# Unit loads ahead of the decay rows' loads, and the first expert's weights split inside the attention units

## The chip, the cores and the metric

The kernel runs on one core of a Trainium2 chip, in one launch. The metric is the device time of that core in microseconds. It is float32 throughout; the large products are made from pairs of rounded halves ("hi" and "lo", type fp32r).

## The reference

Three stages follow each other. B, H, S, D are 2, 8, 768, 40, so that there are 1536 tokens of 320 features.

```python
# 1. gated linear attention, a recurrence over t
m_new = max(f[t] + m, i[t])
f_stab, i_stab = exp(f[t] + m - m_new), exp(i[t] - m_new)
C = f_stab * C + i_stab * outer(v[t], k[t])      # state per batch and head
n = f_stab * n + i_stab * k[t]
y[t] = sigmoid(o[t]) * (C @ q[t]) / max(abs(n . q[t]), 1)
# 2. four dense experts, weights [320, 1024] and [1024, 320]
out += p[:, e] * (relu(x @ w1[e]) @ w2[e])
# 3. eight routed experts, the top one for each token, capacity 384
out[tok] = gate[tok] * (relu(x[tok] @ w1[e]) @ w2[e])
```

## The kernel before

**Attention.** The recurrence is cut into chunks of 128 tokens. A *unit* is one chunk of one batch (8 heads); there are 12, numbered u = 0 to 11, and they alternate between the two batches. For a unit PE (TensorE) makes, in this order: the scores (L445), the first half of the next unit's decay rows spread over 128 partitions (`spread_g`, L432), the products with the carried state (L455), the update of the state (L463), the transposes of the output of unit u-2 (L481), the first three heads' products with v (L473), the second half of the spread (L432), and the other heads' products (L473). ACT (ScalarE) turns the spread rows into `dmat` by Exp (`decays`, L705). POOL (GpSimd) masks a corner of `dmat` (`mask`, L892), weighs v for the next unit (L902), carries the state (`carry_state`, L909), scales the output gate (`scale_o`, L930) and adds up the new state (L918). DVE (VectorE) multiplies scores by `dmat` (`pmat`, L1067), takes the denominator of the unit before (L1103 to L1107), scales `before` (L1077), makes `state_new` (L1083), `x_tok` (L1112) and `xt_lo` (L1118), and at the end `total` (L1095). The order on each engine is written out in the code; semaphores join them.

Waits that matter here: `pmat` of unit u waits for `masked` >= u+1, which POOL's `mask(u)` raises. PE's products with the state of unit u+1 wait for `comb_done`, which DVE's `total` of unit u raises. `scale_o` waits for the reciprocal of the denominator, and `x_tok` for `scale_o`.

**Loads.** SP (SyncE) issues nearly all DMAs, in program order. `load_unit` issues five for a unit: three into `q_diag` (60 KB each), one into `qk_rows` (360 KB) and one into `kv` (324 KB), into four sets of buffers; the load of unit u waits for `in_ready` >= u-3. `load_g` issues one of 8 KB, the decay rows of a unit, two of its partitions only, into two buffers; it waits for `g_spread`, that is until PE has spread the rows of unit u-2.

**Experts' weights.** An expert comes in four pieces p of 704 KB (`load_piece`) into `stage`. ACT rounds a piece into `w1_hi` and `w2_hi` (`w_to_hi`, parts 0 and 1, L737 and L740), DVE makes a shared tail (`w_tail`, L1126), and POOL takes the rests (`w1_to_lo`, L872, which waits for `w_tail`; `w2_to_lo`, L880, which waits for `w_to_hi` part 1). A block of 384 tokens is `up` (L507 to L510) and `down` (L522 to L524). Before, the first expert's piece 0 is loaded after unit 3's load and pieces 1 to 3 after the last unit's; its splitting starts around unit 11 and goes on beside the first block. There `w1_first` and `w_ready` let PE start on the pieces as they are ready.

Of the kernel before, what the change touches and what calls it, by code (L numbers as in the profile page):

```python
# [41 lines left out]
def build_kernel(nc, gates, o_tok, q_t, qk_t, kv_tok, probs, w_moe1, w_moe2, w_gate, out, capacity):  # L42
# [40 lines left out]

    W_STEPS = (1, 3, 5, 7)

    SHIFTED, CHOSEN, SLOTS = 2, 5, 14
# [13 lines left out]
    with ExitStack() as ctx:  # L100
# [174 lines left out]
        w_tail_done = sem("w_tail_done")  # L275
        w1_first = sem("w1_first")
        w_ready = sem("w_ready")
# [30 lines left out]
        def _(sp):  # L308
# [24 lines left out]
            sp.wait_ge(pool_const, CONST_DIAG)  # L333
            load_unit(0, 0)
            sp.wait_ge(g_lo_done, 1)
            sp.dma_start(g_dram.rearrange("n h s -> h n s"), g_split[:].bitcast(F32)).then_inc(g_saved, 16)
            sp.wait_ge(g_saved, 16)
            for b in range(BATCHES):
                sp.wait_ge(mask_rows, b + 1)
                load_g(0, b)  # L340
            load_unit(0, 1)


            for u in range(2, 4):
                sp.wait_ge(g_spread, 2 * (u - 1))
                load_g(u // 2, u % 2)
                load_unit(0, u)
            for p in range(1):
                load_piece(w_moe1, 0, p)
            with sp.Fori(1, UNITS // 4) as i:  # L350
                for j in range(4):
                    sp.wait_ge(in_ready, 4 * i + (j - 3))
                    load_unit(i, j)
                    sp.wait_ge(g_spread, 8 * i + (2 * j - 2))
                    load_g(2 * i + j // 2, j % 2)
            for p in range(1, PIECES):
                load_piece(w_moe1, 0, p)

# [40 lines left out]
        def _(pe):  # L399
# [129 lines left out]
            def first_weights_there(f):  # L529
                if f in LAST_X:  # L530
                    transpose_x(UNITS // 4 - 1, 2 + LAST_X.index(f))
                if f % 2 == 0:
                    pe.wait_ge(w1_first, f // 2 + 1)

            def first_w2_there(n, f):
                if n == 0 and f % 2 == 0:
                    pe.wait_ge(w_ready, f // 2 + 1)
            pe.wait_ge(xt_done, (NT - 1) * BATCHES + 2)
            up(0, 0, lambda k: xt_hi[:, k, 0:BLOCK], lambda k: xt_lo[:, k, 0:BLOCK], first_weights_there)
            down(0, 0, first_w2_there)  # L540

# [141 lines left out]
        def _(act):  # L683
# [40 lines left out]
            decays(0, 2)  # L724
            with act.Fori(0, UNITS // 4 - 1) as i:
                for r in range(2, 6):
                    x_tail(i, r - 2)
                    decays(i, r + 1, [0])
                    x_to_hi(i, r - 2)
                    decays(i, r + 1, [1])  # L730

# [14 lines left out]

            def first_to_hi(p):
                w_to_hi(0, 0, p, 0)
                w_to_hi(0, 0, p, 1)


            i = UNITS // 4 - 1
            x_tail(i, 0)
            decays(i, 3, [0])
            x_to_hi(i, 0)
            decays(i, 3, [1])
            first_to_hi(0)
            x_tail(i, 1)
            x_to_hi(i, 1)
            first_to_hi(1)  # L760
            first_to_hi(2)
            x_tail(i, 2)
            first_to_hi(3)

# [13 lines left out]
            for e in range(E1 - 1):  # L778
                for c in range(BLOCKS1):
                    for f in range(FT):  # L780
                        hidden_hi(BLOCKS1 * e + c, f)

                        if f in ((2, 5) if e or c else (5, 6)):
                            w_to_hi(e + 1, (e + 1) % 2, c, f // 4 if e or c else f - 5)
                        if e == 0 and c == 0:
                            if f + 1 in LAST_X:
                                x_to_hi(UNITS // 4 - 1, 2 + LAST_X.index(f + 1))
                            if f == 1:
                                x_tail(UNITS // 4 - 1, 3)
# [39 lines left out]
        def _(pool):  # L829
# [102 lines left out]


            for u in range(UNITS - BATCHES):
                if u + 1 < UNITS - BATCHES:
                    weigh_v(u + 1)
                    carry_state(u + 1)
                if u:
                    scale_o(u - 1)
                mask(u + 1)  # L940
                new_state(u)
            scale_o(UNITS - 3)
            mask(UNITS - 1)

            for p in range(PIECES):
                w1_to_lo(0, 0, p).then_inc(w1_first, 1)
                if p < 2:
                    scale_o(UNITS - 2 + p)
            for p in range(PIECES):
                w2_to_lo(0, 0, p)  # L950

# [60 lines left out]
        def _(dve):  # L1012
# [133 lines left out]
            attend(0, 1)  # L1146
            with dve.Fori(0, UNITS // 4 - 1) as i:
                for r in range(2, 6):
                    attend(i, r)
            i = UNITS // 4 - 1  # L1150
            attend(i, 2, last_chunk=True)
            w_tail(0, 0, 0, slice(0, PF))
            attend(i, 3, last_chunk=True)
            denominator(i, 3)
            w_tail(0, 0, 1, slice(PF, 2 * PF))
            w_tail(0, 0, 2, slice(2 * PF, 3 * PF))
            w_tail(0, 0, 3, slice(3 * PF, 4 * PF))

# [16 lines left out]
            for f in range(FT):  # L1175
# [3 lines left out]
                if f == 0:  # L1179
                    make_x(UNITS // 4 - 1, 3)  # L1180
                if f == 6:
                    w_tail(1, 1, 0, slice(0, PF))
# [193 lines left out]
```

## Time and profile before

| | |
|---|---|
| median of 3 runs | 634.91 us (634.17 to 637.78) |
| span of the profiled execution, first to last instruction | 634.1 us |
| mean granted TensorE clock over the span | 0.982 |
| PE busy | 588.4 us (93%), 3842 matmuls |
| DVE busy | 285.8 us (45%) |
| ACT busy | 215.3 us (34%) |
| POOL busy | 212.4 us (33%) |

The profiled execution's own time is its span of 634.1 us and what lies around it, 0.8 us if it is like the median run. PE is busy nearly all the time, so the time of the whole is made by PE's work and by the few stretches in which PE has none. Attention's units lie between 23 and 93 us of the span, the first block of the first expert between 93 and 117 us. An engine's low share says nothing about a stage: DVE is busy 45% of the whole, but most of the time in the units.

### The profile page before, as it was taken

To read this page: it belongs to the slowest core of one execution; us is meant where nothing else is said; L and a number is where in the kernel's file an instruction comes from. 1 tells how busy PE (TensorE), PEld (TensorE's weight loads), DVE (VectorE), ACT (ScalarE), POOL (GpSimd) and SP (SyncE) were. 2 spreads that over 40 slices of the span, in tenths; PEclk is the share of its full clock that TensorE was granted. 3 is DMA by queue.
4 is the path that set the end of the run, shared out by engine and by line. 5 is a ranking of instruction groups with operands and counts; after the bars stand their busy time and mean duration, and the time that the engine had idled before them with its cause. 6 is when DMAs were issued, how large, how long until landed. Compare 5 with 4: busy or idle time off the path is not lost.

```text
span 634.1 us, 10634 instructions
## 1 busy us (share of the span) xinstructions
PE 588.4 (93%) x3842; PEld 573.1 (90%) x3842; DVE 285.8 (45%) x607; ACT 215.3 (34%) x468; POOL 212.4 (33%) x238
## 2 busy tenths in 40 slices
PE   0989999999999999999999999999889398899995
PEld 0868889999999999999999999999889398899895
DVE  7268876323332332233223324244425089866362
ACT  5235564212321331133123213214115077646330
POOL 9555539101101110111011011231216157874451
PEclk9999999999999999999999999999979799999999
DMA  6487534941101101110111011120144347774300
GB/s 188 119 207 181 155 152 139 369 190 46 33 12 47 45 3 42 45 47 0 45 45 45 1 47 47 38 81 12 76 141 147 105 136 229 255 231 154 118 15 18
DMA packets 25914, 63.56 MB, mean 100 GB/s; under 512 B 3310, under 2 KB 15543, under 8 KB 25876
## 3 DMA queue, kind: packets, MB, share of 16 engines
q1 hardware_dynamic: 23956, 58.98, 29.3%
q0 software_dynamic: 1920, 4.07, 1.8%
q8 instruction: 25, 0.41, 0.3%
q14 instruction: 13, 0.11, 0.1%
HBM read 52.16 MB, written 13.11 MB: 103 GB/s over the span
## 4 chain that ended last, share of the span: by engine, by line
PE 84%; issue 5%; POOL 3%; DMA 3%; SPq 1%; DVE 1%; ACT 1%; POOLq 0%; DVEq 0%; ACTq 0%
PE bank L507 28%; PE bank L522 12%; PE bank L523 12%; PE bank L524 12%; PE bank L510 5%; PE bank L509 5%; PE bank L445 3%; PE bank L473 2%; DMA g_rows<-g_saved_rows 1%; PE bank L577 1%; PE bank L432 1%; PE bank L636 1%; PE bank L455 1%; PE bank L463 1%; SPq L315 1%
## 5 line engine op out<-in xcount | busy, mean ns | idle before, releaser
L745 ACT ACTIVATE h_hi<-bank 128x384 fp32r<-128x384 f32 x192 | 94.4, 492 | 324.0 <-PE bank L510 323.7
L1161 DVE SCALAR_TENSOR_TENSOR h_lo<-bank,h_hi 128x384 fp32r<-128x384 f32 x192 | 105.5, 556 | 143.4 <-ACT h_hi L745 141.3
L522 PE MATMUL bank<-w_hi_even,h_hi 128*128 128x320 f32 x264 | 81.7, 309 | 0.0
L524 PE MATMUL bank<-w_hi_even,h_lo 128*128 128x320 f32 x264 | 81.6, 309 | 0.0
L523 PE MATMUL bank<-w_lo_even,h_hi 128*128 128x320 f32 x264 | 81.5, 309 | 0.0
L872 POOL TENSOR_TENSOR w_lo_odd<-stage,w_hi_odd 128x512 fp32r<-128x512 f32 x24 | 31.3, 1304 | 149.2 <-DVE w_hi_odd L1126 119.6
L872 POOL TENSOR_TENSOR w_lo_even<-stage,w_hi_even 128x512 fp32r<-128x512 f32 x24 | 31.4, 1308 | 144.2 <-DVE w_hi_even L1126 119.6
L522 PE MATMUL bank<-w_hi_odd,h_hi 128*128 128x320 f32 x248 | 77.4, 312 | 1.4 <-DVE h_lo L1161 1.4
L523 PE MATMUL bank<-w_lo_odd,h_hi 128*128 128x320 f32 x248 | 76.6, 309 | 0.0
L524 PE MATMUL bank<-w_hi_odd,h_lo 128*128 128x320 f32 x248 | 76.6, 309 | 0.0
L507 PE MATMUL bank<-xt_hi,w_hi_odd 128*128 128x384 f32 (+2 forms) x192 | 64.3, 335 | 10.4 <-issue 10.4
L507 PE MATMUL bank<-xt_hi,w_hi_even 128*128 (+2 forms) x192 | 65.2, 339 | 4.8 <-DVE h_lo L1161 1.9
L507 PE MATMUL bank<-xt_lo,w_hi_even 128*128 (+2 forms) x192 | 63.3, 330 | 0.0
L507 PE MATMUL bank<-xt_hi,w_lo_even 128*128 (+2 forms) x192 | 63.2, 329 | 0.0
L1170 DVE SCALAR_TENSOR_TENSOR acc<-bank,prob,acc 128x320 f32 (+1 forms) x36 | 19.8, 551 | 95.8 <-PE bank L524 92.9
L507 PE MATMUL bank<-xt_lo,w_hi_odd 128*128 128x384 f32 (+2 forms) x192 | 62.3, 325 | 0.0
L507 PE MATMUL bank<-xt_hi,w_lo_odd 128*128 128x384 f32 (+2 forms) x192 | 62.3, 324 | 0.0
L522 PEld LDWEIGHTS bank<-w_hi_even,h_hi 128*128 128x128 f32 x264 | 49.6, 188 | 0.3 <-DVE h_lo L1161 0.3
L524 PEld LDWEIGHTS bank<-w_hi_even,h_lo 128*128 128x128 f32 x264 | 49.6, 188 | 0.0
L523 PEld LDWEIGHTS bank<-w_lo_even,h_hi 128*128 128x128 f32 x264 | 49.6, 188 | 0.0
L522 PEld LDWEIGHTS bank<-w_hi_odd,h_hi 128*128 128x128 f32 x248 | 46.6, 188 | 1.7 <-DVE h_lo L1161 1.7
L523 PEld LDWEIGHTS bank<-w_lo_odd,h_hi 128*128 128x128 f32 x248 | 46.6, 188 | 0.0
(162 smaller groups left out, 1165.8 us busy)
## 6 DMA issues: line engine op xcount, KB each, us to landing
stage<-w_moe SPq DMA_DIRECT2D x48, 704.0 KB, 4.0
slot_rows<-empty_row SPq DMA_DIRECT2D x1, 4632.0 KB, 20.0
x_slot<-slot_rows SPq DMA_DIRECT2D x24, 193.0 KB, 3.9
qk_rows<-qk_t SPq DMA_DIRECT2D x12, 360.0 KB
kv<-kv_tok SPq DMA_DIRECT2D x12, 324.0 KB
q_diag<-q_t SPq DMA_DIRECT2D x36, 60.0 KB
sig<-o_tok SPq DMA_DIRECT2D x2, 960.0 KB, 6.8
out<-empty_row SPq DMA_DIRECT2D x2, 960.0 KB, 18.6
```

What stands on the lines that cost most here:

```text
L445: pe.matmul(ps_s[g][:, lo:IN_GROUP * P], qk_rows[j][:, 1, g, :], q_diag[j][:, g, lo:], start=True, stop=True).then_inc(s_ready, 1)
L473: mm = pe.matmul(ps_in[:, h * V1:(h + 1) * V1], pmat[:, h, :], v41[j][:, h, :], start=True, stop=True)
L507: pe.matmul(dst, wk[w][:, k, cols], xk(k), start=(n == 0), stop=False)
L509: pe.matmul(dst, w1_hi[w][:, 2, cols], xh(2), start=False, stop=False)
L510: pe.matmul(dst, w1_hi[w][:, 2, cols], xl(2), start=False, stop=True).then_inc(h_psum, 1)
L522: pe.matmul(ps_y[n][:, 0:X], h_hi[:, f, rows], w2_hi[w][:, f, :], start=(f == 0), stop=False)
L523: pe.matmul(ps_y[n][:, 0:X], h_hi[:, f, rows], w2_lo[w][:, f, :], start=False, stop=False)
L524: mm = pe.matmul(ps_y[n][:, 0:X], h_lo[:, f, rows], w2_hi[w][:, f, :], start=False, stop=(f == FT - 1))
L745: act.activation(h_hi[:, f, :], ps_h[f % 3][:, 0:BLOCK], ACT.Relu).then_inc(h_hi_done, 1)
L872: return pool.tensor_tensor(w1_lo[w][:, :, cols], raw1[:, 0:2, :], w1_hi[w][:, 0:2, cols].bitcast(F32), ALU.subtract)
L1161: dve.scalar_tensor_tensor(h_lo[:, f, :], ps_h[f % 3][:, 0:BLOCK], 0.0, h_hi[:, f, :].bitcast(F32), ALU.max, ALU.subtract).then_inc(h_done, 1)
L1170: op = dve.scalar_tensor_tensor(acc[:, tile, 0:X], ps_y[n][:, 0:X], share, acc[:, tile, 0:X], ALU.mult, ALU.add)
```

## The change

SP's loads of the first four units move ahead of the decay rows' loads. The loop over the other units is written out, and a piece of the first expert is loaded behind the decay rows of units 4, 5, 6 and 7. In the units from 4 on, ACT rounds one part of a piece per unit, DVE makes a piece's tail behind each even unit, and POOL takes one rest per unit: w1's in the even ones, w2's in the odd ones. `w1_first` is gone; PE waits for `w_ready` alone. For the second expert, ACT rounds its first piece behind tiles 2 and 5 of the first block, not behind 5 and 6.

```diff
 (SP)
-            load_unit(0, 0)
+            for j in range(2):
+                load_unit(0, j)
             sp.wait_ge(g_lo_done, 1)
...
                 load_g(0, b)
-            load_unit(0, 1)
+            for j in range(2, 4):
+                load_unit(0, j)
             for u in range(2, 4):
                 sp.wait_ge(g_spread, 2 * (u - 1))
                 load_g(u // 2, u % 2)
-                load_unit(0, u)
-            for p in range(1):
-                load_piece(w_moe1, 0, p)
...
+            for u in range(4, UNITS):
+                sp.wait_ge(in_ready, u - 3)
+                load_unit(u // 4, u % 4)
+                sp.wait_ge(g_spread, 2 * (u - 1))
+                load_g(u // 2, u % 2)
+                if u >= FIRST_W and u < FIRST_W + PIECES:
+                    load_piece(w_moe1, 0, u - FIRST_W)
 (ACT)
+            for u in range(2, UNITS - 1):
+                x_tail(0, u - 2)
+                decays(0, u + 1, [0])
+                x_to_hi(0, u - 2)
+                decays(0, u + 1, [1])
+                if u >= FIRST_W:
+                    w_to_hi(0, 0, (u - FIRST_W) // 2, (u - FIRST_W) % 2)
...
+            w_to_hi(0, 0, PIECES - 1, 1)
             x_tail(i, 2)
-            first_to_hi(3)
 (POOL)
                 if u:
                     scale_o(u - 1)
+                if u >= FIRST_W:
+                    first_to_lo(u - FIRST_W)
                 mask(u + 1)
                 new_state(u)
             scale_o(UNITS - 3)
+            first_to_lo(UNITS - 2 - FIRST_W)
             mask(UNITS - 1)
-            for p in range(PIECES):
-                w1_to_lo(0, 0, p).then_inc(w1_first, 1)
-                if p < 2:
-                    scale_o(UNITS - 2 + p)
-            for p in range(PIECES):
-                w2_to_lo(0, 0, p)
+            first_to_lo(UNITS - 1 - FIRST_W)
+            scale_o(UNITS - 2)
+            scale_o(UNITS - 1)
 (DVE)
+            for u in range(2, UNITS):
+                attend(0, u, last_chunk=u >= UNITS - BATCHES)
+                if u >= FIRST_W and u % 2 == 0:
+                    p = (u - FIRST_W) // 2
+                    w_tail(0, 0, p, slice(p * PF, (p + 1) * PF))
```

The order on SP, from the first unit's load to the load of unit 4, before. `g_saved_rows` is where the decay rows lie in DRAM.

```order
L315 DMA q_diag<-q_t 40x3x128 x3
L316 DMA qk_rows<-qk_t 120x768
L317 DMA kv<-kv_tok 128x648
L321 DMA g_rows<-g_saved_rows 2x8x128 [waits g_spread]
L315 DMA q_diag<-q_t 40x3x128 x3
L316 DMA qk_rows<-qk_t 120x768
L317 DMA kv<-kv_tok 128x648
L324 DMA stage<-w_moe 128x1408
```

These rows are unit 2's load, the decay rows of unit 3, unit 3's load and the first piece; unit 4's load follows. The same place after:

```order
L316 DMA q_diag<-q_t 40x3x128 x3
L317 DMA qk_rows<-qk_t 120x768
L318 DMA kv<-kv_tok 128x648
L322 DMA g_rows<-g_saved_rows 2x8x128 [waits g_spread] x2
L316 DMA q_diag<-q_t 40x3x128 [waits in_ready]
L316 DMA q_diag<-q_t 40x3x128 x2
L317 DMA qk_rows<-qk_t 120x768
L318 DMA kv<-kv_tok 128x648
L322 DMA g_rows<-g_saved_rows 2x8x128 [waits g_spread]
L325 DMA stage<-w_moe 128x1408
```

Unit 3's load now stands ahead of the decay rows of units 2 and 3, and the first piece behind the load and the decay rows of unit 4.

The order on POOL in a unit, before; `dmat` in the fourth row is the mask of the next unit.

```order
L902 TENSOR_TENSOR vw<-kv,cols 128x328 [waits upd_ready,unit_in1]
L909 TENSOR_TENSOR state_kept<-state,c_all 120x369 [waits state_done]
L930 TENSOR_TENSOR osc<-sig,rden 128x320 [waits x_main,rden_done]
L892 AFFINE_SELECT dmat<-dmat 2x8x2 [waits exp_done]
L918 TENSOR_TENSOR state<-state_new,state_kept 120x369 [waits state_step,state_carried]
```

And after, in units 4 and 5:

```order
L888 TENSOR_TENSOR vw<-kv,cols 128x328 [waits upd_ready,unit_in1]
L895 TENSOR_TENSOR state_kept<-state,c_all 120x369 [waits state_done]
L916 TENSOR_TENSOR osc<-sig,rden 128x320 [waits x_main,rden_done]
L858 TENSOR_TENSOR w_lo_even<-stage,w_hi_even 128x2x256 [waits w_tail_done]
L878 AFFINE_SELECT dmat<-dmat 2x8x2 [waits exp_done]
L904 TENSOR_TENSOR state<-state_new,state_kept 120x369 [waits state_step,state_carried]
L888 TENSOR_TENSOR vw<-kv,cols 128x328 [waits upd_ready,unit_in2]
L895 TENSOR_TENSOR state_kept<-state,c_all 120x369 [waits state_done]
L916 TENSOR_TENSOR osc<-sig,rden 128x320 [waits x_main,rden_done]
L866 TENSOR_TENSOR w_lo_even<-stage,w_hi_even 128x640 [waits w_hi_done]
L878 AFFINE_SELECT dmat<-dmat 2x8x2 [waits exp_done]
```

A rest of the weights now stands between `scale_o` and the next unit's mask. The last rows of POOL's part in attention, before and after:

```order
L892 AFFINE_SELECT dmat<-dmat 2x8x2 [waits exp_done]
L872 TENSOR_TENSOR w_lo_even<-stage,w_hi_even 128x2x256 [waits w_tail_done]
L930 TENSOR_TENSOR osc<-sig,rden 128x320 [waits x_main,rden_done]
L872 TENSOR_TENSOR w_lo_even<-stage,w_hi_even 128x2x256 [waits w_tail_done]
L930 TENSOR_TENSOR osc<-sig,rden 128x320 [waits x_main,rden_done]
L872 TENSOR_TENSOR w_lo_even<-stage,w_hi_even 128x2x256 [waits w_tail_done] x2
L880 TENSOR_TENSOR w_lo_even<-stage,w_hi_even 128x640 [waits w_hi_done] x4
```

Behind unit 11's mask there were four rests of w1 and four of w2. After:

```order
L916 TENSOR_TENSOR osc<-sig,rden 128x320 [waits x_main,rden_done]
L858 TENSOR_TENSOR w_lo_even<-stage,w_hi_even 128x2x256 [waits w_tail_done]
L878 AFFINE_SELECT dmat<-dmat 2x8x2 [waits exp_done]
L866 TENSOR_TENSOR w_lo_even<-stage,w_hi_even 128x640 [waits w_hi_done]
L916 TENSOR_TENSOR osc<-sig,rden 128x320 [waits x_main,rden_done] x2
```

Now the last rest of w1 stands ahead of unit 11's mask, and one rest of w2 behind it.

## Rows read from the trace of the kernel before

**Rows 1.** The page: the span, and TensorE's busy time.

```profile
span 634.1 us, 10634 instructions
PE 588.4 (93%) x3842; PEld 573.1 (90%) x3842; DVE 285.8 (45%) x607; ACT 215.3 (34%) x468; POOL 212.4 (33%) x238
```

**Rows 2.** Timeline, PE: scores of units 3, 4, 10, 11 (start, duration in us).

```profile
41.75 1.97 PE L445 MATMUL bank<-q_diag,qk_rows 120*128 120x384 f32 x6
...
50.44 1.97 PE L445 MATMUL bank<-q_diag,qk_rows 120*128 120x384 f32 x6
...
84.02 1.97 PE L445 MATMUL bank<-q_diag,qk_rows 120*128 120x384 f32 x6
...
88.95 1.97 PE L445 MATMUL bank<-q_diag,qk_rows 120*128 120x384 f32 x6
```

**Rows 3.** Chain that ended last, 36 to 52 us: start, duration, what.

```profile
39.06 7.36 DMA g_rows<-g_saved_rows
46.42 0.12 issue
46.54 0.50 PE bank L432
```

**Rows 4.** Timeline, SP: when DMAs are issued.

```profile
24.70 0.28 SPq L321 DMA_DIRECT2D g_rows<-g_saved_rows  x1
...
34.12 0.43 SPq L324 DMA_DIRECT2D stage<-w_moe  x1
...
34.92 2.74 SPq L315 DMA_DIRECT2D q_diag<-q_t  x3
...
38.43 0.36 SPq L317 DMA_DIRECT2D kv<-kv_tok  x1
```

**Rows 5.** Timeline, PE and POOL in unit 8.

```profile
73.30 0.23 POOL L892 TENSOR_SCALAR_AFFINE_SELECT dmat<-dmat 2x16 f32<-2x16 f32 x1 [1.70 <-ACT dmat L705]
...
74.86 0.79 PE L455 MATMUL bank<-state,qk_rows 120*128 120x123 f32 x6
75.14 0.79 POOL L909 TENSOR_TENSOR state_kept<-state,c_all 120x369 f32<-120x369 f32 x1
...
76.48 0.76 PE L473 MATMUL bank<-kv,pmat 128*128 128x41 f32 x6
```

**Rows 6.** Timeline, DVE in unit 8: `pmat`, `den`, `total`.

```profile
73.75 1.53 DVE L1067 TENSOR_TENSOR pmat<-bank,dmat 128x384 f32<-128x384 f32 x3 [0.22 <-PE bank L445]
...
75.20 0.76 DVE L1103 SCALAR_TENSOR_TENSOR den<-total 128x8 f32<-128x8 f32 x1
...
78.63 0.49 DVE L1095 TENSOR_TENSOR total<-before,bank 128x328 f32<-128x328 f32 x1 [0.40 <-PE bank L473]
```

**Rows 7.** Timeline, unit 11 and the first block's start, DVE and POOL.

```profile
90.02 0.42 DVE L1126 TENSOR_TENSOR w_hi_even<-stage,w_hi_even 64x256 fp32r<-64x256 f32 x1 [0.37 <-ACT w_hi_even L737]
...
90.53 1.27 POOL L872 TENSOR_TENSOR w_lo_even<-stage,w_hi_even 128x512 fp32r<-128x512 f32 x1 [0.97 <-DVE w_hi_even L1126]
...
91.75 0.16 DVE L1103 SCALAR_TENSOR_TENSOR den<-total 128x8 f32<-128x8 f32 x1
...
97.99 2.80 POOL L872 TENSOR_TENSOR w_lo_even<-stage,w_hi_even 128x512 fp32r<-128x512 f32 x2
98.42 1.22 DVE L1112 TENSOR_TENSOR x_tok<-total,osc 128x320 f32<-128x320 f32 x1
...
100.75 6.14 POOL L880 TENSOR_TENSOR w_lo_even<-stage,w_hi_even 128x640 fp32r<-128x640 f32 x4
```

**Rows 8.** Stretches: each engine's busy us (x instructions), PE clock, DMA share, GB/s.

```profile
34.00:40.00 6.00, 6.00 (x46) 5.34 (x44) 4.93 (x14) 2.75 (x11) 3.63 (x6) 1.00 0.91 272
40.00:52.00 12.00, 9.18 (x61) 7.63 (x61) 6.93 (x17) 4.80 (x16) 4.86 (x8) 1.00 0.93 189
```

**Rows 9.** Stretches again: the first block, and a later one for comparison.

```profile
93.39:117.03 23.64, 23.33 (x145) 22.43 (x145) 11.77 (x23) 9.11 (x19) 15.20 (x18) 1.00 0.58 191
138.70:160.36 21.66, 21.66 (x137) 21.66 (x137) 6.54 (x12) 5.28 (x10) 2.88 (x2) 1.00 0.10 34
```

More of the change, by code:

```diff
@@ L84, in build_kernel @@
     W_STEPS = (1, 3, 5, 7)
+    FIRST_W = 4
     SHIFTED, CHOSEN, SLOTS = 2, 5, 14
@@ L275, in build_kernel @@
         w_tail_done = sem("w_tail_done")
-        w1_first = sem("w1_first")
         w_ready = sem("w_ready")
@@ L346, in _ @@
                 load_g(u // 2, u % 2)
-                load_unit(0, u)
-            for p in range(1):
-                load_piece(w_moe1, 0, p)
[L350 to L357, printed above, removed]
+            for u in range(4, UNITS):
[5 more added lines that the diff above has]
+                    load_piece(w_moe1, 0, u - FIRST_W)
             for p in range(PIECES):
@@ L532, in first_weights_there @@
                 if f % 2 == 0:
-                    pe.wait_ge(w1_first, f // 2 + 1)
-            def first_w2_there(n, f):
-                if n == 0 and f % 2 == 0:
                     pe.wait_ge(w_ready, f // 2 + 1)
@@ L539, in _ @@
             up(0, 0, lambda k: xt_hi[:, k, 0:BLOCK], lambda k: xt_lo[:, k, 0:BLOCK], first_weights_there)
-            down(0, 0, first_w2_there)
+            down(0, 0)
             pe.wait_ge(xt_done, UNITS + 1)
@@ L724, in _ @@
             decays(0, 2)
[L725 to L730, printed above, removed]
             def w_to_hi(x, w, p, part):
@@ L745, in hidden_hi @@
                 act.activation(h_hi[:, f, :], ps_h[f % 3][:, 0:BLOCK], ACT.Relu).then_inc(h_hi_done, 1)
-            def first_to_hi(p):
-                w_to_hi(0, 0, p, 0)
-                w_to_hi(0, 0, p, 1)
-            i = UNITS // 4 - 1
[L753 to L757, printed above, removed]
+            for u in range(2, UNITS - 1):
[5 more added lines that the diff above has]
+                    w_to_hi(0, 0, (u - FIRST_W) // 2, (u - FIRST_W) % 2)
+            i = UNITS // 4 - 1
             x_tail(i, 1)
             x_to_hi(i, 1)
-            first_to_hi(1)
-            first_to_hi(2)
+            w_to_hi(0, 0, PIECES - 1, 1)
             x_tail(i, 2)
-            first_to_hi(3)
             def yt_to_sbuf(t):
@@ L781, in _ @@
                         hidden_hi(BLOCKS1 * e + c, f)
-                        if f in ((2, 5) if e or c else (5, 6)):
-                            w_to_hi(e + 1, (e + 1) % 2, c, f // 4 if e or c else f - 5)
+                        if f in (2, 5):
+                            w_to_hi(e + 1, (e + 1) % 2, c, f // 4)
                         if e == 0 and c == 0:
@@ L931, in scale_o, with first_to_lo @@
                                    rden[:].unsqueeze(2).broadcast_to([P, HEADS, D]), ALU.mult).then_inc(osc_done, 1)
+            def first_to_lo(step):
+                p = step // 2
+                if step % 2 == 0:
+                    w1_to_lo(0, 0, p)
+                else:
+                    w2_to_lo(0, 0, p)
             for u in range(UNITS - BATCHES):
@@ L1146, in _ @@
             attend(0, 1)
-            with dve.Fori(0, UNITS // 4 - 1) as i:
-                for r in range(2, 6):
-                    attend(i, r)
+            for u in range(2, UNITS):
[3 more added lines that the diff above has]
+                    w_tail(0, 0, p, slice(p * PF, (p + 1) * PF))
             i = UNITS // 4 - 1
-            attend(i, 2, last_chunk=True)
-            w_tail(0, 0, 0, slice(0, PF))
-            attend(i, 3, last_chunk=True)
             denominator(i, 3)
-            w_tail(0, 0, 1, slice(PF, 2 * PF))
-            w_tail(0, 0, 2, slice(2 * PF, 3 * PF))
-            w_tail(0, 0, 3, slice(3 * PF, 4 * PF))
             def hidden_lo(g, f):
@@ L1180, in _ @@
                     make_x(UNITS // 4 - 1, 3)
-                if f == 6:
+                if f == 3:
                     w_tail(1, 1, 0, slice(0, PF))
```

## The prediction

> **What bounds the kernel now.** I read the page first: PE is busy 93% of the span [rows 1], so an edit off PE counts only where PE waits for it. The change touches the attention units and the first block, so I read the timeline there. From unit 4 on the scores start every 5.60 us, (84.02 - 50.44) / 6 [rows 2], and PE is busy throughout: a unit is PE's own work. One step is longer: 8.69 us from unit 3 to unit 4 [rows 2]. The chain of waits names the cause: the decay rows of unit 4 are issued at 39.06 and land 7.36 us later, and the spread starts at 46.54 [rows 3]. SP was late, since it issued unit 3's load, the first piece (34.12) and unit 4's load (34.92 to 38.79) first [rows 4]. Then I read one unit on DVE and POOL, for what they can take in [rows 5, 6], and the first block against a later one [rows 9].
>
> I write T for the start of a unit's scores. For unit 8, whose rows are shown, T = 84.02 - 2 x 5.60 = 72.82.
>
> **Part 1, the loads.** The decay rows of unit 4 may be issued once unit 2's are spread, near 35.4, and only unit 4's load is then ahead of them: with the 4 us or so that a row behind one load should need they land near 40, and PE wants them at T+1.7, near 43.4. The step of 8.69 becomes 5.60: **-3.1 us**. The price: the decay rows of unit 2 were issued at 24.70 [rows 4]; now one load more precedes them, 3.9 us of SP's time at most (34.92 to 38.79), so they are issued near 28.1 to 28.6. Behind one load in flight such a row should take some 4 us (less than the 7.36 behind a load and a piece [rows 3]), so it lands near 32.4 to 32.9, and PE wants it near 32.5 (two steps of some 5.4 before 41.75, and 1.7). **+0.2**, bounds 0 and 0.5. Unit 1's early load runs while the queue is empty and SP idle: nothing.
>
> **Part 2, the split.** All weight work is moved, none added: 4 tails at 0.42 us, 4 rests of w1 at 1.27, 4 of w2 at 6.14 / 4 = 1.54 [rows 7]. What counts is its place. POOL's mask(u+1) now stands behind the rest of w1, this behind DVE's tail, and this behind `total`(u).
>
> Natural unit: mask at T+0.47 to 0.70, `pmat` at T+0.92, PE's state products at T+2.03, its first v products at T+3.65 [rows 5, 6]. So `pmat` has 3.65 - 0.92 - 0.5 (its first third) = 2.2 us of cover, and `total`(u-1), which ends at T+0.70, has 1.3.
> - Link A, `total` end to `pmat` in an even-to-odd step: tail 0.42, 0.09 to POOL (90.44 to 90.53), rest 1.27, mask 0.23, some 0.1 of handing over: 2.15 us, where 0.22 was.
> - Link B, `pmat` start to `total` end: 78.63 - 0.40 of waiting + 0.49 - 73.75 = 4.95 [rows 6]. It holds the 0.6 us by which `den` takes 0.76 beside POOL's `carry_state`, and 0.16 where POOL is idle [rows 5 to 7]; units 9 to 11 have no `carry_state` beside it, so B is 4.1 there.
> - Link C, odd-to-even: the rest of w2 can start once `scale_o` is through, near T+0.9 to 1.1, and takes 1.54; mask and `pmat` follow at T+3.2. That is within PE's cover, but later than the 0.22 after `total`.
>
> I follow them unit by unit. With the stall gone T4 = 47.55, T5 = 53.15. For unit 5 the tail waits for ACT's rounding until T+1.2 (as at 90.02 [rows 7]), so `pmat` starts at T5+3.4 and its first third is out at T5+3.9: PE is 0.3 late, T6 = 59.05. `total`(5) ends at T5+3.4+4.9 = T6+2.4; PE wants it at about T+1.8: 0.6 late. T7 = 65.25. Unit 6's `pmat` at T6+3.2 is in time, its `total` ends at T7+1.9 (0.15 late), and A puts unit 7's `pmat` at T7+4.05, its first third at T7+4.55: 0.8 more. T8 = 71.8. From here it repeats: T9 = 78.05, T10 = 84.55. A pair of units takes 12.7 us, and A + B + 0.75 + B is 2.15 + 4.95 + 0.75 + 4.95 = 12.8; PE alone needs 11.2. Unit 10 (B = 4.1) costs 0.55 over its 4.93 us [rows 2]: T11 = 90.05. Unit 11 is worst, since a last unit has no state update to give cover: its first v products were at T+2.7, and `pmat` now comes at T+3.75, so they wait 1.5 us. The first block starts at 96.05, where it was 93.39: **+2.65** in all, that is -3.1 + 0.2 + (0.3 + 1.55 + 1.55 + 0.55 + 1.5).
>
> **Part 3, the first block.** It took 23.64 us, a later one 21.66 [rows 9]; two sets of transposes explain 0.7, so 1.3 was waiting for weights and for an ACT blocked by the second expert's first piece. These waits go. But `scale_o` of unit 10 now stands behind a rest of w2, so unit 10's transposes come about 0.8 late. Net **-0.5**, bounds -1.3 and +0.5. PE's code and everything later is as before.
>
> **Sum:** -3.1 + 0.2 + 5.45 - 0.5 = +2.05 us. On the profiled execution 634.1 becomes 636.2; with the 0.8 around it, against a median of 634.91, **637.0 us**.
>
> **A rule weighed against the trace.** `den` takes 0.16 us with POOL idle and 0.76 beside `carry_state`, and `x_tok` took 1.22 us when it began 0.43 after a rest of w1 [rows 5 to 7]; both end as POOL's instruction ends. The Trainium skill, "SBUF — State Buffer", section "Who interferes with whom", says that a VectorE operation with two SBUF inputs and a GpSimd one that reads SBUF exclude each other for a whole instruction, by who issues first. The trace agrees with it. By the rows alone I take `x_tok` to go ahead of the rest, which is 637.0; by the rule it hangs on 0.1 us of order, and the other outcome is the second rival, 638.5.
>
> **The rivals.**
> 1. *The cover holds* (0.15). If links A to C are shorter than I make them, or DVE catches up, only -3.1 + 0.2 - 0.5 to -1.3 is left: 631.5, down to 630.7. For it: PE needs none of this work before T+2. Against: A alone takes 1.9 of the 2.2 us, in front of a chain that is already 4.95 of 5.60.
> 2. *`x_tok` loses to the rest of w2* (0.20). In an odd-to-even step both are ready within 0.2 us, near T+0.95. If POOL starts first, `x_tok` waits 1.54 and `total` ends at T+3.8, not 2.4. PE loses 1.45 in that unit, and 0.7 comes back since the next mask is earlier: 0.75 for each of two pairs, 638.5.
> 3. *The DMA queue becomes the bound* (0.15, slower). A unit's load and a piece are 0.885 + 0.72 = 1.6 MB per unit, from unit 5 to 8. At 272 GB/s that takes 5.9 us, at 189 GB/s 8.5 [rows 8]; I take the middle, 7.2. Unit 4's load lands near 38.4; the decay rows of unit 8, behind four such pairs, land at 38.8 + 4 x 7.2 = 67.6, and PE wants them at T7+1.6 = 66.85. The 0.75 lies inside the wait for `pmat` of unit 7. So it decides from 7.2 us a pair on; at 8.0 the rows come at 70.8, 3.2 after that point, 640 us.
> 4. *The stall of unit 4 stays* (0.04), for the queue and not SP makes the rows late: 640.
>
> **How the numbers follow.** My forecast, 637.0, has 0.40, with 635.5 to 638.0 as its own range; 0.06 is left for what I don't see. What a measurement can tell from no change is about 0.5%, 3.2 us: below 631.7 is faster, above 638.1 slower. Faster takes the better half of rival 1: 0.09. Slower takes half of rival 2, most of 3, 4, and the forecast's upper end: 0.33. The rest, 0.58, is the same. The range is 633.0 to 641.0: it leaves out most of rival 1 and little above.
>
> **What would show it.** Right, if in the profile after: the scores' step from unit 3 to 4 is 5.6 us with no wait of the spread for a DMA; the steps from unit 5 to 10 are about 6.2 to 6.5; POOL's longest waits there are for DVE's tail and DVE's for POOL's mask; the first v products of unit 11 wait for `pmat`; the first block starts 2 to 3 us later and takes about 23.1. Wrong, if steps stay at 5.6 (rival 1), `x_tok` takes 1.2 us or more in odd units (2), PE's spread waits for `g_rows` in units 6 to 8 (3) or in unit 3 (4).

## The result, and the profile after

The changed kernel took 649.24 us, the median of 4 runs (644.03 to 654.71), against 635.49 us for the kernel before on the same chip: ratio 1.0173, 95% interval 1.0113 to 1.0233. The ratio leaves out the run of 654.71 us, which was in a slower state (its mean granted clock was 0.956, against 0.963 to 0.976 in the others), while the medians hold all runs. The kernel is slower, by more than twice what the upper end of the forecast range allowed. Measured again it took 649.94 us, with a ratio of 1.0219 (1.0174 to 1.0264).

The page of its profiled execution, which was the fastest of the four runs: the span and TensorE's busy time, to be read against [rows 1].

```profile
span 642.2 us, 10358 instructions
PE 592.3 (92%) x3842; PEld 575.5 (90%) x3842; DVE 286.3 (45%) x607; ACT 216.3 (34%) x468; POOL 212.7 (33%) x238
```

The number of products is the same and the span 8.1 us longer. The timeline of PE in this execution (start, duration, in brackets the idle time ahead and who ended it) answers to [rows 2].

```profile
23.74 3.61 PE L444 MATMUL bank<-q_diag,qk_rows 120*128 120x384 f32 x6
...
42.15 1.97 PE L444 MATMUL bank<-q_diag,qk_rows 120*128 120x384 f32 x6
47.75 1.97 PE L444 MATMUL bank<-q_diag,qk_rows 120*128 120x384 f32 x6
...
59.06 1.97 PE L444 MATMUL bank<-q_diag,qk_rows 120*128 120x384 f32 x6
62.97 0.87 PE L454 MATMUL bank<-state,qk_rows 120*128 120x123 f32 x6 [1.71 <-DVE total L1088]
66.60 1.97 PE L444 MATMUL bank<-q_diag,qk_rows 120*128 120x384 f32 x6
...
83.14 0.86 PE L472 MATMUL bank<-kv,pmat 128*128 128x41 f32 x6 [0.62 <-DVE pmat L1060]
85.18 3.26 PE L444 MATMUL bank<-q_diag,qk_rows 120*128 120x384 f32 x6
91.78 1.97 PE L444 MATMUL bank<-q_diag,qk_rows 120*128 120x384 f32 x6
95.45 1.98 PE L472 MATMUL bank<-kv,pmat 128*128 128x41 f32 x16 [0.75 <-DVE pmat L1060]
```

A unit's step is the time from its scores to those of the next unit, formed from unrounded starts. The step from unit 3 to unit 4 is 5.60 us, where it was 8.69: the stall is gone. From unit 6 on PE waits for `total` and `pmat`, as the links A to C have it. The wait of 0.62 us is followed by scores of 3.26 us rather than 1.97: PE's granted clock was 0.50 from 85.7 to 89.1. The chain of waits, in place of [rows 3], shows unit 2's decay rows:

```profile
28.14 4.79 DMA g_rows<-g_saved_rows
32.93 0.04 issue
32.98 0.49 PE bank L431
```

They are issued at 28.14 and land 4.79 us later, as forecast, and PE's spread is 0.4 us late: unit 1 takes 5.68 us where 5.27 is PE's own.

This execution flatters the change. In the profile of the second set of runs, PE's full clock was granted 10 us earlier, at 17.7 us of the span rather than 27.7. The clock column of the views counts the time ahead of the first grant as full, so this is read from the lengths of PE's products: unit 0's scores took 1.88 us rather than the 3.61 above. Unit 0 took 5.90 us rather than 7.13, and everything behind it is another picture. PE's timeline there:

```profile
21.23 1.88 PE L444 MATMUL bank<-q_diag,qk_rows 120*128 120x384 f32 x6
...
27.13 1.97 PE L444 MATMUL bank<-q_diag,qk_rows 120*128 120x384 f32 x6
32.88 0.80 PE L431 MATMUL bank<-g_rows,spread_w 128*128 128x512 f32 x1 [3.78 <-DMA g_rows<-g_saved_rows]
...
39.68 3.76 PE L444 MATMUL bank<-q_diag,qk_rows 120*128 120x384 f32 x6
47.88 1.97 PE L444 MATMUL bank<-q_diag,qk_rows 120*128 120x384 f32 x6
...
68.69 0.87 PE L454 MATMUL bank<-state,qk_rows 120*128 120x123 f32 x6 [1.71 <-DVE total L1088]
...
81.97 0.87 PE L454 MATMUL bank<-state,qk_rows 120*128 120x123 f32 x6 [1.72 <-DVE total L1088]
```

SP's issues in the same profile, and three stretches of it (the column before the DMA share is the granted clock, as a share of full speed):

```profile
24.71 2.39 SPq L316 DMA_DIRECT2D q_diag<-q_t  x3
...
28.13 0.58 SPq L322 DMA_DIRECT2D g_rows<-g_saved_rows  x2
```

```profile
27.00:31.40 4.40, 2.10 (x9) 1.17 (x8) 2.88 (x7) 0.44 (x2) 3.34 (x5) 1.00 0.93 241
31.40:45.00 13.60, 12.12 (x44) 10.45 (x45) 3.93 (x10) 3.53 (x13) 3.13 (x6) 0.50 0.57 161
45.00:60.00 15.00, 15.00 (x108) 13.37 (x108) 11.78 (x27) 8.15 (x28) 6.93 (x11) 1.00 0.79 233
```

SP is no earlier than in the other execution: the decay rows of unit 2 go out at 28.13 behind unit 3's load, where it was 28.14. PE wants them at 29.1 and has nothing to do for 3.78 us. From 31.4 to 45.0 it is then granted 0.50 of full speed, that is 1.2 GHz rather than 2.4. The steps of units 1 and 2 become 12.55 and 8.20 us, where PE needs 5.27 and 5.59.

### The profile page after: what moved, and what is told of

Its sections match the earlier page's. It is cut to its first block, busy times and chain, and to the rows that moved or that the text cites. A ratio compares the mean times of both kernels' runs of the same rounds, so it can differ in the third digit from the quotient of the medians.

```text
span 642.2 us, 10358 instructions
## 1 busy us (share of the span) xinstructions
PE 592.3 (92%) x3842; PEld 575.5 (90%) x3842; DVE 286.3 (45%) x607; ACT 216.3 (34%) x468; POOL 212.7 (33%) x238
## 3 DMA queue, kind: packets, MB, share of 16 engines
q1 hardware_dynamic: 23956, 58.98, 29.1%
## 4 chain that ended last, share of the span: by engine, by line
PE 80%; issue 6%; DVE 5%; POOL 4%; DMA 2%; ACT 1%; SPq 1%; POOLq 0%; DVEq 0%; ACTq 0%
PE bank L506 28%; PE bank L521 12%; PE bank L523 12%; PE bank L522 12%; PE bank L509 5%; PE bank L508 5%; DVE pmat L1060 1%; PE bank L573 1%; PE bank L472 1%; PE bank L444 1%; PE bank L632 1%; DVE den L1096 1%; PE bank L562 1%; POOL c_select L828 1%; DMA g_rows<-g_saved_rows 1%
## 5 line engine op out<-in xcount | busy, mean ns | idle before, releaser
L858 POOL TENSOR_TENSOR w_lo_odd<-stage,w_hi_odd 128x512 fp32r<-128x512 f32 x24 | 31.4, 1308 | 153.6 <-DVE w_hi_odd L1119 124.0
L506 PEld LDWEIGHTS bank<-xt_hi,w_hi_odd 128*128 128x128 f32 x192 | 36.9, 192 | 14.1 <-issue 12.5
```

The costliest lines, as they stand in the source:

```text
L506: pe.matmul(dst, wk[w][:, k, cols], xk(k), start=(n == 0), stop=False)
L858: return pool.tensor_tensor(w1_lo[w][:, :, cols], raw1[:, 0:2, :], w1_hi[w][:, 0:2, cols].bitcast(F32), ALU.subtract)
```

## The experiments

Three things were to be told apart: the late decay rows (with the clock behind them), the split inside the units, and the pieces on the DMA queue. The table gives what was measured; the last column, from the first scores of unit 1 to the first block of the first expert, is read from PE's timeline in each profile. A profile is of one execution, the medians are of all. The kernels were measured in three sets, each on a chip of its own and with the kernel before beside them: its medians were 636.15 us (changed again, loads alone, mask ahead, rests later), 635.42 (rows first, loads alone and changed; gap filled, loads alone) and 636.47 (gap filled, changed; pieces later). Across sets the ratios are the fairer measure.

| kernel | median, us | ratio to before (95%) | steps of units 1, 2 | unit 1 to first block |
|---|---|---|---|---|
| before, profiled again | 637.32 (1 run) | | 6.98, 5.59 | 61.15 |
| changed, again | 649.94 | 1.0219 (1.0174 to 1.0264) | 12.55, 8.20 | 75.46 |
| loads alone | 639.10 | 1.0053 (1.0022 to 1.0084) | 10.57, 8.11 | 67.26 |
| mask ahead of the rest | 641.21 | 1.0081 (1.0052 to 1.0111) | 10.75, 7.92 | 67.26 |
| rests a unit later | 643.83 | 1.0123 (1.0092 to 1.0153) | 12.26, 7.09 | 71.11 |
| rows first, loads alone | 636.47 | 1.0028 (1.0003 to 1.0053) | 5.27, 5.59 | 62.52 |
| rows first, changed | 641.85 | 1.0088 (1.0060 to 1.0116) | 5.27, 5.59 | 68.41 |
| gap filled, loads alone | 632.07 | 0.9956 (0.9933 to 0.9980) | 8.46, 5.59 | 62.62 |
| gap filled, changed | 639.11 | 1.0036 (1.0009 to 1.0062) | 8.46, 5.59 | 68.86 |
| rows first, pieces later | 633.47 | 0.9963 (0.9937 to 0.9988) | 5.27, 5.59 | 59.44 |

**The changed kernel again.** No edit. 

> The changed kernel as it is, for more runs and a second profile. Order theory (POOL's rest of the weights ahead of the mask, and the exclusion of x_tok by that rest): the first block starts 3 to 5 us later than before (93.4) in every run, 96 to 98 us, with the same two links; this part is about +4 us and no more. Clock theory, for what lies above that: the runs differ by more than 5 us among themselves, and their time falls with the granted clock of the run; stretches at the half clock level lie behind gaps of PE. If the order theory alone held, runs would agree within 1 us near 639 to 640.

The loss is the same as at first, and the profile is the one shown above. The runs differ by 9.7 us and the granted clock falls from 0.971 in the shortest to 0.955 in the longest, as the clock theory has it; the first block starts at 102.59 and not by 98, since the late rows stand ahead of it. From unit 4 on its steps are 5.59, 5.71, 7.55, 5.72, 7.55, 5.71 and 5.43 us.

**Loads alone.** The changed order on SP in full, with the split on ACT, DVE and POOL as before. 

> SP's order as in the changed kernel (unit loads ahead, a piece behind the decay rows of units 4 to 7), the splitting and all else as before. Order theory: the step from unit 3 to 4 is 5.6 us, all steps to unit 10 are 5.6, the first block starts at 90.3 to 90.8 and the time is 632.0 to 633.0. DMA theory (pieces beside unit loads fill the queue): steps of units 5 to 8 exceed 6 us and the spread waits for g_rows there; time 635 or more. Clock: as before, within 1 us, if the splitting causes the losses.

PE's timeline and a stretch of this profile:

```profile
27.74 1.97 PE L445 MATMUL bank<-q_diag,qk_rows 120*128 120x384 f32 x6
32.31 0.50 PE L432 MATMUL bank<-g_rows,spread_w 128*128 128x512 f32 x1 [2.60 <-DMA g_rows<-g_saved_rows]
38.31 3.76 PE L445 MATMUL bank<-q_diag,qk_rows 120*128 120x384 f32 x6
46.42 1.97 PE L445 MATMUL bank<-q_diag,qk_rows 120*128 120x384 f32 x6
```

```profile
33.00:45.00 12.00, 12.00 (x56) 10.42 (x54) 4.99 (x13) 3.70 (x14) 3.34 (x5) 0.57 0.64 184
```

A wait of 2.60 us, and then 0.57 of the clock, by themselves: the loads, forecast to gain 2.9 us, lose 0.5%. All steps from unit 3 to unit 10 are 5.6 us, so the pieces cost nothing here. The runs of this kernel fall into two groups by the mean clock that each was granted: five at 0.967 to 0.972 took 640.7 to 644.1 us, six at 0.976 to 0.981 took 636.2 to 639.1. The profile is of the first group; what the second looks like in units 1 and 2 is not shown.

**Mask ahead of the rest.** The changed kernel, with POOL's `mask` and `new_state` first and the rest of the weights behind them.

```diff
-                if u >= FIRST_W:
-                    first_to_lo(u - FIRST_W)
                 mask(u + 1)
                 new_state(u)
+                if u >= FIRST_W:
+                    first_to_lo(u - FIRST_W)
...
```

> The changed kernel with POOL's mask(u+1) and new_state(u) ahead of the rest of the weights, in units 4 to 11. Order theory: link A leaves the path; pmat starts 1.6 us after the scores in odd units and not 3.4, the steps are 5.6 to 5.8, the first block starts at 90.5 to 92, time 632 to 634. If the exclusion of VectorE by POOL's rest is the main cost, den and x_tok still take over 1 us and the steps stay at 6 or more: 637 or more. If the DMA queue is the cause, nothing changes: 644 or more.

All steps from unit 3 to unit 10 are 5.6 us, and the last column is that of loads alone to the hundredth. So the whole price of the split in the units comes through one order, the rest ahead of the mask. The order holds two things that this run doesn't part: `pmat` no longer waits behind the rest, and the rest no longer lies beside `x_tok`, which takes 0.49 us in every unit. Against the changed kernel in the same set this gives back 8.7 us of median; the late rows remain, and with them the time is 641.21 and not the 632 to 634 expected. The first block gains nothing from weights that are ready. It takes 24.0 us, for PE meets the wait below at its second set of transposes (timeline of PE):

```profile
97.89 0.52 PE L480 MATMUL bank<-ident,x_tok 128*128 128x128 f32 x3 [1.43 <-DVE xt_lo L1111]
```

**Rests a unit later.** The changed kernel, POOL's rests each one unit later, so that none waits for DVE's tail of its own unit.

```diff
-                if u >= FIRST_W:
-                    first_to_lo(u - FIRST_W)
+                if u >= FIRST_W + 1:
+                    first_to_lo(u - FIRST_W - 1)
                 mask(u + 1)
...
```

> The changed kernel with each rest one unit later on POOL, at the same place ahead of the mask, so that the rest's inputs are ready before its turn. Order theory: POOL no longer waits there for DVE's tail, and the mask is on time; what is left is the exclusion: x_tok, ready with the rest, takes up to 1.3 to 1.5 us more in each unit, total comes 1.5 us after the scores and not 0.7, within PE's cover; steps 5.6 to 6.0, first block at 91 to 93, 632.5 to 635. If exclusion is the main cost instead, all steps are 6.2 or more and the time is over 638.

The steps of units 5 to 8 are 5.96, 6.25, 6.44 and 6.27. The jagged 5.7 and 7.55 are gone, but POOL's rests still stand ahead of the mask, and PE's waits are 0.42, 0.43 and 0.36 us for `total`, instead of 1.7, and one of 0.55 for `pmat`. Of the split's 6.1 us 3.2 remain: waiting for the tail was only a part of the price. What remains is POOL's rest beside DVE's work. The two in unit 6 (POOL and DVE):

```profile
63.89 1.27 POOL L858 TENSOR_TENSOR w_lo_even<-stage,w_hi_even 128x512 fp32r<-128x512 f32 x1
63.96 1.54 DVE L1106 TENSOR_TENSOR x_tok<-total,osc 128x320 f32<-128x320 f32 x1
```

From unit 6 to unit 11 `x_tok` takes 1.54 to 1.82 us each time, not 0.49, and `total` comes after it.

**Before, profiled again.** No edit, one run. 

> The kernel before, for a second profile. The runs so far show two starts: the clock is granted at 27.7 us and unit 0's scores begin at 23.7, or it is granted at 17 to 20 us and they begin at 21.2 to 21.9. Rows theory (the decay rows of unit 2, issued behind three unit loads, are late): with an early clock this kernel, which issues them at 24.7, shows a wait of under 0.5 us there, no half clock in the units before 100 us, a stall of 3 to 5 us at unit 4, and a first block at 92 to 94. If the loss seen in the four last profiles belongs to the early clock itself, this kernel shows a wait of 2.6 us or more in unit 1 and half clock from 31 to 45 us as well.

PE's timeline, to be held against [rows 2]:

```profile
28.57 3.68 PE L445 MATMUL bank<-q_diag,qk_rows 120*128 120x384 f32 x6 [1.20 <-DMA kv<-kv_tok]
35.55 1.97 PE L445 MATMUL bank<-q_diag,qk_rows 120*128 120x384 f32 x6
41.14 1.97 PE L445 MATMUL bank<-q_diag,qk_rows 120*128 120x384 f32 x6
46.74 1.97 PE L445 MATMUL bank<-q_diag,qk_rows 120*128 120x384 f32 x6
```

Here, too, the clock came early, and the picture on which the forecast rested is not there: the step from unit 3 to 4 is 5.60, with no stall to remove. The decay rows of unit 4 are issued at 38.01, and PE doesn't wait for them when it comes to them near 42.8, so they landed within 4.8 us rather than 7.36. Instead PE waits 1.20 us for unit 1's load, and its scores take 3.68 us at the lower clock level. The granted clock is 0.50 from 28.6 to 32.0. That is what unit 1's earlier load can take away. One profile of each sort says nothing on how often either occurs.

**Rows first, loads alone.** Loads alone, but the decay rows of units 2 and 3 are issued ahead of their units' loads, as before the change; unit 1's load stays early.

```diff
-            for j in range(2, 4):
-                load_unit(0, j)
             for u in range(2, 4):
                 sp.wait_ge(g_spread, 2 * (u - 1))
                 load_g(u // 2, u % 2)
+                load_unit(0, u)
```

> The kernel e1 with the decay rows of units 2 and 3 issued ahead of the loads of these units, the splitting as before. Rows theory: the rows of unit 2 are issued near 21.5 us and land by 24; no wait of the spread for them, no half clock between 28 and 45 us, steps of 5.3 to 5.9 up to unit 4 and 5.6 behind it; the first block starts at 87.5 to 90.5, and the time is 4 to 7 us below that of e1, 632 to 634. If the wait has another cause (the DMA queue, full of unit loads), the rows still land at 29 or later, and the time stays near 639.

No wait in units 1 and 2 and no lower clock before 455 us of the span. But the third rival now shows (timeline of PE, units 5 to 7):

```profile
51.58 0.50 PE L429 MATMUL bank<-g_rows,spread_w 128*128 128x512 f32 x1 [0.41 <-DMA g_rows<-g_saved_rows]
58.63 0.50 PE L429 MATMUL bank<-g_rows,spread_w 128*128 128x512 f32 x1 [1.19 <-DMA g_rows<-g_saved_rows]
65.16 0.50 PE L429 MATMUL bank<-g_rows,spread_w 128*128 128x512 f32 x1 [0.67 <-DMA g_rows<-g_saved_rows]
```

The steps there are 6.27, 7.05 and 6.53: with PE some 8 us further on, the queue of a load and a piece per unit is too slow by 3.1 us in all. In the kernel with loads alone the stall of units 1 and 2 had covered this.

**Rows first, changed.** The same edit of SP's order in the changed kernel. 

> The changed kernel with the decay rows of units 2 and 3 issued ahead of the loads of these units; the splitting as in the changed kernel. Rows theory: 6 to 9 us less than the changed kernel, and no half clock at 31 to 45 us. Order theory for what is left against e5: units 5 to 10 still take 6 to 7.5 us each where POOL's rest stands ahead of the mask, the first block starts 5 to 8 us later than in e5, and the time is 638 to 643. If the chain of rests costs nothing once the clock holds, it is within 1.5 us of e5.

It gives back a good half of the loss, 1.0219 to 1.0088 (two sets of runs on different chips), and is still slower than before. Its longest waits are one of 2.09 us for `g_rows` in unit 5, which is the third rival again, and 0.63 and 1.13 for `pmat`; the split costs 68.41 - 62.52 = 5.9 us against the kernel above, with a lower clock from 54.5 to 57.9, behind the wait of 2.09, in it.

**Gap filled, loads alone.** The late rows stay, but PE has something to do while it waits: 56 products of constants, 128 by 128 (bf16), into a buffer that nobody reads then, between unit 1's scores and the spread. Nothing else is changed.

```diff
-            def keep_warm(products, left, right):
+            def keep_warm(products, left, right, dst=ps_before):
...
+                if isinstance(i, int) and i == 0 and r == 1:
+                    keep_warm(56, ones[:], tri[:], ps_t)
```

> The kernel e1 with 56 small products on PE (bf16, 128x128, into a bank that nobody reads) between unit 1's scores and the spread that waits: 3 us of work at the full clock, where PE sat idle 2.6 us. The rows' lateness is unchanged. Clock theory: the idle gap is what lets the clock fall, so the clock stays at its full level from 28 to 45 us, the step from unit 1 to 2 is 8 to 9 us (10.6 in e1) and from 2 to 3 5.6 to 6 (8.1); the first block starts 3.5 to 5 us earlier than in e1 and the time is 3 to 5 us less. If the fall has another cause, the half clock comes at 31 to 35 us all the same and the time is that of e1 or up to 1 us more.

PE's timeline, and the stretch that was at 0.57 of the clock in loads alone:

```profile
28.02 1.97 PE L445 MATMUL bank<-q_diag,qk_rows 120*128 120x384 f32 x6
29.82 3.29 PE L403 MATMUL bank<-tri,ones 128*128 128x128 bf16 x56
...
36.47 1.97 PE L445 MATMUL bank<-q_diag,qk_rows 120*128 120x384 f32 x6
42.07 1.97 PE L445 MATMUL bank<-q_diag,qk_rows 120*128 120x384 f32 x6
```

```profile
33.00:45.00 12.00, 12.00 (x87) 10.63 (x86) 8.56 (x19) 5.87 (x21) 5.80 (x9) 1.00 0.83 253
```

The rows are no earlier than before: they are issued at 29.16, where it was 28.10, and the idle products take the place of the wait, so that unit 1 takes 8.46 us rather than 5.27. But the clock stays, unit 2 takes 5.59, and the median falls from 639.10 to 632.07 (ratios 1.0053 and 0.9956, again in two sets). No run of this kernel was granted less than 0.978. In the units of the two profiles the late rows cost 7.8 us, 2.60 of them the wait itself; with the filling the price is 3.2, the idle products' own time. More than half of the price is not the wait but the clock behind it. The gain of 7.0 us of median is more than the 3 to 5 expected.

**Gap filled, changed.** The same products in the changed kernel. 

> The changed kernel with the same 56 small products that fill PE's wait for unit 2's decay rows in the gap-filled loads-alone kernel (632.07). Theory (two separate costs, the clock's fall behind the late rows and the split's chain): no half clock at units 1 to 3, steps of 8.5 and 5.6 there, later steps as in the changed kernel (5.7 to 7.5), and a time that is 632.1 plus the chain's price, 5.45 - 0.5 as forecast plus up to 2 for half clock at its own waits: 637 to 639. Rival (the chain alone costs what parts the changed kernel from loads alone, 649.9 - 639.1 = 10.8): 642 to 643. Rival (nearly all is the clock's fall behind the rows): 633 to 634.

The median is 639.11, where without the filling it was 649.94. What is left over the kernel with loads alone and the gap filled is the split by itself: 639.11 - 632.07 = 7.0 us of median, 0.8% or 5.1 us by the ratios, and 68.86 - 62.62 = 6.2 us in the units of the two profiles. PE's longest waits there:

```profile
65.83 0.87 PE L456 MATMUL bank<-state,qk_rows 120*128 120x123 f32 x6 [1.72 <-DVE total L1090]
79.09 0.87 PE L456 MATMUL bank<-state,qk_rows 120*128 120x123 f32 x6 [1.72 <-DVE total L1090]
...
97.90 2.13 PE L474 MATMUL bank<-kv,pmat 128*128 128x41 f32 x16 [1.12 <-DVE pmat L1062]
```

**Rows first, pieces later.** Rows first with loads alone, the pieces behind the decay rows of units 6, 8, 10 and 11.

```diff
-                if u >= FIRST_W and u < FIRST_W + PIECES:
-                    load_piece(w_moe1, 0, u - FIRST_W)
+                if u in PIECE_UNITS:        # (6, 8, 10, 11)
+                    load_piece(w_moe1, 0, PIECE_UNITS.index(u))
```

> The rows of the decay first, unit 1's load early, the split where it was before, and the four pieces loaded behind units 6, 8, 10 and 11 rather than 4 to 7. Theory (the queue is the bound where a piece lies behind every unit, which cost the rows-first kernel steps of 6.27, 7.05 and 6.53 us rather than 5.59): no wait of the spread for the decay rows in any unit, every step of the scores from unit 2 on 5.6 us, the first block near 87.2 (89.66 less the 3.1 us over in those steps, or up to 0.7 later if the pieces are short for the first block), and the time 636.5 - 3 = 633.5, between 632 and 635. Rival (the rows are late for another reason than the pieces): the steps of units 5 to 7 stay near 6.3 to 7, 636.5.

Every step from unit 1 on is PE's own work, with no wait for `g_rows` and no lower clock in the units. The first block starts at 86.63, 3.03 us earlier than with rows first alone, which is the 3.1 us of the three steps. It is faster than before, at 0.9963; it and the kernel with loads alone and the gap filled (0.9956) beat both kernels, and are not told apart, the less so as they were measured in different sets.

## Why the prediction was wrong

**The loads, -3.1 and +0.2: the step that failed.** The forecast put the decay rows of unit 2 at 0.2 us, "bounds 0 and 0.5". The issue at 28.1 to 28.6 and the landing 4 us or so later were right (28.13 to 28.14, and 4.79). What failed was the moment at which PE wants them, "near 32.5". That came from one execution, in which PE's clock was granted late (from 27.7 of the span) and unit 0 took 7.17 us. In nine of the ten profiles of the experiments it is granted between 17.7 and 20.3. PE then wants the rows at 29.1 to 29.7 and, in the four profiles where the rows stand behind unit 3's load and nothing fills the wait, waits 2.59 to 3.78 us. In the changed kernel that costs 12.55 - 5.27 + 8.20 - 5.59 = 9.9 us in units 1 and 2. The wait itself is 3.78 of it, and the other 6.1 lie behind it, where the clock is 0.50. The forecast has no term for the clock at all: it priced a late row by its lateness alone. The same execution gave the -3.1: before, profiled again, has no stall at unit 4. The forecast saw the condition, the rows' landing against PE's arrival, but took PE's side of it as fixed; its bounds were made from SP's side alone. In the fastest of the first four runs, whose profile had the late clock, its numbers for these rows held (PE was 0.4 us late), which is why that profile alone would not have shown the failure.

**Unit 1's early load, "nothing": mis-sized the other way.** With the early clock it takes away 1.20 us of waiting and a lower clock behind it, 6.98 - 5.27 = 1.7 us in unit 1 and 7.27 - 5.90 = 1.4 in unit 0. The kernel with the rows first and the pieces later gains 0.4%, 3.0 us of median, and these 3.1 us would account for it; no run moves unit 1's load alone.

**The split, +5.45: right in mechanism and nearly in size.** With no lower clock behind a late row the two kernels with the gap filled differ by 6.2 us up to the first block. The forecast had 5.45, and 6.95 with its second rival in both pairs of units, which is what happened there. Unit 11's loss, put at 1.5, shows in the gap-filled pair: the step from unit 11 to the first block is 5.97 us with the split and 4.47 without, 1.5 more. In the profile after, which had the late clock of the forecast's own execution, the forecast's starts can be laid beside the measured ones: unit 4 at 47.55 and 47.75, unit 6 59.05 and 59.06, unit 7 65.25 and 66.60, unit 8 71.80 and 72.32, unit 10 84.55 and 85.18, unit 11 90.05 and 91.78, the first block 96.05 and 97.26. (Unit 10 holds the lower clock from 85.7, which the forecast doesn't have.) Link A can be seen in unit 7 (DVE and POOL), the second rival in units 6 and 8:

```profile
59.32 0.72 POOL L916 TENSOR_TENSOR osc<-sig,rden 128x320 f32<-128x320 f32 x1 [0.55 <-DVE rden L1100]
60.07 1.54 POOL L866 TENSOR_TENSOR w_lo_even<-stage,w_hi_even 128x640 fp32r<-128x640 f32 x1
60.08 1.88 DVE L1105 TENSOR_TENSOR x_tok<-total,osc 128x320 f32<-128x320 f32 x1
...
66.81 0.50 DVE L1088 TENSOR_TENSOR total<-before,bank 128x328 f32<-128x328 f32 x1
67.68 0.42 DVE L1119 TENSOR_TENSOR w_hi_even<-stage,w_hi_even 64x256 fp32r<-64x256 f32 x1 [0.37 <-ACT w_hi_even L727]
68.18 1.28 POOL L858 TENSOR_TENSOR w_lo_even<-stage,w_hi_even 128x512 fp32r<-128x512 f32 x1 [2.46 <-DVE w_hi_even L1119]
69.41 0.23 POOL L878 TENSOR_SCALAR_AFFINE_SELECT dmat<-dmat 2x16 f32<-2x16 f32 x1
69.67 1.35 DVE L1060 TENSOR_TENSOR pmat<-bank,dmat 128x384 f32<-128x384 f32 x3 [1.57 <-POOL dmat L878]
...
73.34 0.49 DVE L1105 TENSOR_TENSOR x_tok<-total,osc 128x320 f32<-128x320 f32 x1
73.34 1.90 POOL L866 TENSOR_TENSOR w_lo_even<-stage,w_hi_even 128x640 fp32r<-128x640 f32 x1
```

From the end of `total` at 67.31 to `pmat` at 69.67 it is 2.36 us, forecast 2.15 (its parts add up to 2.11). The tail's wait of 0.37 for ACT is what the forecast didn't have; the handings-over are shorter than it made them. At 60.08 `x_tok` stood beside POOL's rest, began 0.01 us after it and took 1.88 us; at 73.34 it took 0.49, and the rest took 1.90 instead of 1.54. This is the second rival, and it fell one way or the other within the same execution. The Trainium skill, "SBUF — State Buffer", section "Who interferes with whom", says that the two exclude each other for a whole instruction by who issues first. The trace agrees with it that one waits for the other; who issued first it doesn't show, for the records of the two begin within 0.01 us of each other both times. One reading of the forecast was off here: `x_tok` at 98.42 [rows 7] ended at 99.64, not with POOL's first rest, which ended at 99.28, but 0.36 us behind it, as if its own work began then. Where `x_tok` lost, the unit took 7.55 us and the next 5.72, together 13.27, where the forecast had 12.7 and its rival 13.45. In the changed kernel again and with the gap filled it lost in both units 6 and 8 (1.86 to 1.88 us), and both took 7.55; here unit 8, where it won, took 6.16.

**The first block, -0.5: no gain.** From its first product to that of the next block it took 23.60 us in the profile after, where it was 23.45 before, and 23.9 to 24.0 in the changed kernel again and with the gap filled, with 3.4 us of lower clock in each. The 1.3 us of waiting that the forecast took away was hardly there: PE was busy for 23.33 of the 23.64 us [rows 9]. In its place PE waits for `xt_lo`, 1.00 us in the profile after and 1.43 with the mask ahead. In the profile after the bound of +0.5 held.

**The third rival** (the DMA queue) does not show in the changed kernel, whose other waits put PE later, and costs 3.1 us where these are taken away. **The first** (the cover holds) fell: only with the mask ahead of the rest is it so.

**The sum.** The forecast's terms ahead of the first block add up to 2.55 and not to the 2.65 it gives; nothing hangs on it. From unit 1 to the first block the changed kernel needs 75.46 us, and 59.44 are PE's own: 9.9 + 6.1 = 16.0 over. The medians of this kernel and of the one with the rows first and the pieces later differ by 649.94 - 633.47 = 16.5, or 16.3 by the ratios, since they are from different sets. The kernel before was itself 1.7 + 1.4 over in its early-clock profile, which leaves 12.9, against the measured 13.8.

What stays open: first, why the full clock is granted at 18 or at 28 us of the span from one execution to the next. Second, the routed stage, whose code is the same in all kernels, took 161.2 to 168.7 us in the twelve profiles, and 4 of the 8.1 us of the profile after lie in it; the two profiles of the kernel before have 163.2 and 168.7, so no part of this is put down to the change. Third, filling the wait gave back 10.8 us of median in the changed kernel and 7.0 with loads alone (11.6 and 6.2 by the ratios), where the units of the profiles account for 6.6 and 4.6. The two kernels with the gap filled have the shortest routed stages of all, 161.2 and 161.9; whether the filling has a part in that was not tested.

## What to carry to other kernels

Before you cost a reordered load at nothing, work out when its consumer can want it in the fastest execution, not only in the profiled one: a queue that runs by itself doesn't become earlier when the engine does. Where TensorE must wait some microseconds, look at its clock behind the wait: here idle products in the wait (ratio 0.9956) did as much as taking the wait away (0.9963, with the pieces later). Put work that has slack behind the small instruction that others wait for (here a mask of 0.23 us), not ahead of it, and look at what it lies beside on the other engines.

## What the runs showed of the hardware

The granted clock followed the waits of PE near the start. A wait of 2.6 to 3.8 us at 29 to 33 us of the span was followed by 10 to 14 us at 0.50 of full speed, the wait of 1.20 in the kernel before by 3.4 us; with the wait filled there was none at this place. The Trainium skill, "TensorE: Matmul & The Clock Gate", section "HAM oscillation — how this bites in real kernels", tells of kernels in which TensorE waits for a DMA and starts again at the lower clock; the trace agrees. The length of a wait doesn't decide alone: the 2.8 us ahead of 46.54 [rows 3] and the waits of 1.7 us in the changed kernel were followed by no lower clock; the 2.09 us in rows first, changed, the 1.12 us ahead of the first block in the changed kernel again and with the gap filled, and the 0.62 us ahead of 83.14 by 3.4 us of it each. The 1.13 us ahead of the first block in rows first, changed, were followed by none there.

The same program, the changed kernel, was granted its full clock at 17.7 and at 27.7 us of the span in two executions, which moves what PE does there against what the DMA queues do.
